# Attention and two MLP stages on one core: the seven-sum form of the second product in 19 of 24 blocks

## What is computed

```
q_n, k_n = rmsnorm(q, g_q), rmsnorm(k, g_k)
attn = softmax(q_n @ k_n^T / sqrt(64));  x = (attn @ v) as (4, 448, 768)
xn = (x - mean) / sqrt(var + 1e-6) * g_ln
x = x + relu(xn @ w_ch1) @ w_ch2             # first MLP
u = x + (x^T @ U @ V)^T                      # mixing over the sequence, rank 32
out = u + relu(u @ w_ch1b) @ w_ch2b          # second MLP
```

## Time and profile before

| | before |
|---|---|
| median of 3 runs | 1674.16 us |
| the profiled execution | 1675.43 us, span 1673.6 us |
| granted TensorE clock, mean | 0.998 |
| TensorE matmul busy | 98% of the span, 9878 instructions |
| VectorE, ScalarE, GpSimd busy | 68%, 44%, 29% |
| DMA | 43% of 16 engines' time, 146 GB/s |

### The profile page before, as it was taken

One profiled execution on the slowest core, in us unless ns is written; L12 is line 12 of the kernel. 1 busy time (PEld: TensorE's weight loads), 2 busy tenths in 40 slices (PEclk: granted clock), 3 DMA queues, 4 the chain that ended last, 5 costly groups with the idle time before them and its releaser, 6 DMA issues.

```text
span 1673.6 us, 27323 instructions
## 1 busy us (share of the span) xinstructions
PE 1632.0 (98%) x9878; PEld 1452.8 (87%) x9878; DVE 1140.2 (68%) x1934; ACT 736.8 (44%) x1637; POOL 482.8 (29%) x426
## 2 busy tenths in 40 slices
PE   9999988899999999999999999999999999999998
PEld 7766666688999999998899999999999899999998
DVE  6877788865556558838766787556645783766667
ACT  5777887852333224413433343323323431443333
POOL 5666777811111114201220132111111330122211
PEclk9999999999999999999999999999999999999999
DMA  4223333223555356452355355445535754234541
GB/s 124 73 66 89 88 121 117 84 86 116 183 179 188 126 193 215 167 192 93 129 181 185 121 190 186 164 143 175 186 122 179 254 188 150 81 123 161 170 169 68
DMA packets 92308, 243.68 MB, mean 146 GB/s; under 512 B 10160, under 2 KB 41008, under 8 KB 92176
## 3 DMA queue, kind: packets, MB, share of 16 engines
q1 hardware_dynamic: 92176, 241.94, 43.3%
HBM read 162.07 MB, written 79.82 MB: 145 GB/s over the span
## 4 chain that ended last, share of the span: by engine, by line
PE 78%; DVE 2%; ACT 1%; DMA 1%; issue 1%; SPq 0%; DVEq 0%; ACTq 0%
PE mm_ps L1002 35%; PE mm_ps L1021 26%; PE mm_ps L1011 12%; PE mm_ps L956 1%; PE sc_ps L1033 1%; PE sc_ps L1043 1%; PE sc_ps L943 1%; PE mm_ps L935 1%; PE sc_ps L977 1%; DMA w_kept<-w_hl 0%; DVE acc L1432 0%; PE sc_ps L1051 0%; ACT e_t L1120 0%; DVE h_lo L1396 0%; DVE w_hl L1360 0%
## 5 line engine op out<-in xcount | busy, mean ns | idle before, releaser
L1002 PE MATMUL mm_ps<-in_hi,w_hl 128*128 128x448 f32 x2016 | 589.5, 368 | 1.2 <-DVE ht L1417 1.1
L1021 PE MATMUL mm_ps<-h_hi,w_hl 128*128 128x448 f32 x1440 | 417.2, 367 | 0.0
L1002 PEld LDWEIGHTS mm_ps<-in_hi,w_hl 128*128 128x128 f32 x2016 | 379.0, 188 | 32.3 <-issue 2.0
L1002 PE MATMUL mm_ps<-in_lo,w_hl 128*128 128x448 f32 x1008 | 368.9, 366 | 0.0
L1021 PEld LDWEIGHTS mm_ps<-h_hi,w_hl 128*128 128x128 f32 x1440 | 270.7, 188 | 22.4
L1021 PE MATMUL mm_ps<-h_lo,w_hl 128*128 128x448 f32 x720 | 263.7, 366 | 0.0
L1157 ACT ACTIVATE w_hl<-w_raw 128x384 fp32r<-128x384 f32 (+1 forms) x382 | 173.1, 469 | 157.1 <-PE mm_ps L1021 78.0
L1441 DVE TENSOR_TENSOR acc<-mm_ps,acc 128x448 f32<-128x448 f32 x180 | 103.8, 618 | 201.0 <-PE mm_ps L1021 200.9
L1011 PE MATMUL mm_ps<-h_hi,w_hl 128*128 128x448 f32 x756 | 220.9, 367 | 0.5 <-issue 0.5
L1002 PEld LDWEIGHTS mm_ps<-in_lo,w_hl 128*128 128x128 f32 x1008 | 189.7, 188 | 14.7
L1360 DVE TENSOR_TENSOR w_hl<-w_raw,w_hl 128x384 fp32r<-128x384 f32 (+1 forms) x382 | 194.3, 517 | 5.0 <-ACT w_hl L1157 4.5
(11 more groups left out here) (119 smaller groups left out, 2289.1 us busy)
## 6 DMA issues: line engine op xcount, KB each, us to landing
w_raw<-in_w SPq DMA_DIRECT2D x76, 768.0 KB, 5.4
w_kept<-w_hl SPq DMA_DIRECT2D x140, 384.0 KB, 6.3
w_hl<-w_kept SPq DMA_DIRECT2D x140, 384.0 KB, 3.9
qk<-in_qkv SPq DMA_DIRECT2D x23, 448.0 KB, 4.1
acc<-xres SPq DMA_DIRECT2D x6, 1344.0 KB, 9.8
qt_raw<-in_q_t SPq DMA_DIRECT2D x24, 224.0 KB, 2.9
v<-in_qkv SPq DMA_DIRECT2D x24, 224.0 KB, 2.6
xnrm<-st_n SPq DMA_DIRECT2D x24, 224.0 KB, 2.0
```

The source lines that it names most:

```text
L1002: last = nc.tensor.matmul(bank(q), w[a][:, c * P:(c + 1) * P], x[:, k, c], start=k not in ONTO and c == 0 and p == 0, stop=c == HC - 1 and ...
L1021: last = nc.tensor.matmul(bank(q, b), w[a][:, c * P:(c + 1) * P], x[:, half, 2 * c + b], start=half == 0 and c == 0 and p == 0, stop=half ...
```

## The change

1. `by_sums` becomes true in 19 blocks: `SUMS_FROM = (2, 0, 0, 0)`, that is j = 2 to 4 of stage 0, j = 0 to 4 of stages 1 and 2, and j = 0 to 5 of stage 3. Which groups' weights are stored and fetched (`FIRST_KEPT = 1`) stays, so in the 10 added blocks the first product's weights are split in the block itself.
2. A third buffer `w_raw2`, used from block 2 of stage 0 on (its first load stands at product 42); buffers are taken in turn.
3. The differences for P7 and P4 move from VectorE to GpSimd (`later_sum`, with the semaphore `sub2_done`); that of P7 stands at m0 + 1 instead of m0 + 2.
4. Positions: G weights are split 4 instead of 3 products ahead from group 2 of stage 0; S weights 6 ahead where the block's groups are fetched, 5 where they are split; the sums of weights move along. P2 is split at m0 + 6 and P4 at m0 + 9. Stores of split weights stand 3 products earlier in the DMA queue's order.
5. Mixing: one item per 24 products in both stages, the same offsets for both. Inputs of a next stage are loaded at -13, -8 and 2 in all stages.

```diff
-    FIRST_KEPT, FLIP = 1, 0
+    FIRST_KEPT, SUMS_FROM, THIRD_FROM = 1, (2, 0, 0, 0), 42
     def by_sums(s, j):
-        return s % 2 == 1 and FIRST_KEPT <= j and (s == STAGES - 1 or j < NJ - 1)
+        return SUMS_FROM[s] <= j and (s == STAGES - 1 or j < NJ - 1)
...
-        high_at.setdefault(q - (7 if kind == "S" else 4), []).append(q)
-        low_at.setdefault(q - (6 if kind == "S" else 3), []).append(q)
+        low_lead[q] = 4 if kind == "G" and q >= number["G", 0, 2, P1] else 3 if kind != "S" else 6 if kept(number["G", s, 2 * n, P1]) else 5
+        high_at.setdefault(q - low_lead[q] - 1, []).append(q)
+        low_at.setdefault(q - low_lead[q], []).append(q)
...
-            sums_at.setdefault(number["G", s, n, P1] + {P5: -5, P7: -5, P6: -4, P3: 0}[k], []).append(q)
+            sums_at.setdefault(number["G", s, n, P1] + {P5: -5, P7: -5, P6: -4, P3: 0}[k] + 3 - low_lead[q], []).append(q)
         if kind == "S" and k[0] in (P5, P7, P6, P3):
-            sums_at.setdefault(q - {P5: 11, P7: 16, P6: 9, P3: 9}[k[0]], []).append(q)
+            first = {P5: 11, P7: 16, P6: 9, P3: 9} if low_lead[q] == 6 else {P5: 9, P7: 14, P6: 9, P3: 8}
+            sums_at.setdefault(q - first[k[0]], []).append(q)
...
+        third = run[0] >= number["G", 0, 2 * SUMS_FROM[0], P1]
+        x = min(range(2 + third), key=lambda x: loaded[x][-1:] or [-1])
...
-                                (P7, m0 + 2, m0 + 4), (P2, None, m0 + 5), (P4, m0 + 6, m0 + 8)):
+                                (P7, m0 + 1, m0 + 4), (P2, None, m0 + 6), (P4, m0 + 6, m0 + 9)):
...
-    MIX_FROM, MIX_STEP, ITEMS = 4, {1: 23, 2: 22}, 2 * HC
+    MIX_FROM, MIX_STEP, ITEMS = 4, 24, 2 * HC
...
+                def later_sum(s, j, k):
+                    g = s * NG + 2 * j
+                    if k == P7:
+                        rectified(pool, g + 1, C12)
+                        cut(pool, "f", s, j, P5)
+                        in0, in1 = relu_pair(g + 1, SECOND), relu_pair(g, SECOND)
+                    if k == P4:
+                        rectified(pool, g + 1, C21)
+                        cut(pool, "f", s, j, P6)
+                        in0, in1 = relu_pair(g + 1, FIRST), sub_pair(P6)
+                    nc.gpsimd.tensor_tensor(sub_pair(k), in0, in1, ALU.subtract).then_inc(sub2_done, 1)
...
-                        if stored(n):
-                            store_split(n)
+                        if n + 3 < Q and stored(n + 3):
+                            store_split(n + 3)
```

More of the change, by code:

```diff
@@ L103, in planned @@
         at = dict(zip(ks, at))[k[0] if kind == "S" else k]
-        at = at if j % 2 == FLIP else (at + 3) % 6
+        if j == SUMS_FROM[s] and kind == "G" and n % 2 == 0 and k == P1:
+            flip[s] = j % 2 if free.index(0) < free.index(3) else 1 - j % 2
+        at = at if j % 2 == flip[s] else (at + 3) % 6
         return [at + d for d in range(HC)] if kind == "S" else [at]
     banks, before = {}, {}
-    free, last_use = list(range(6)), {}
+    free, last_use, flip = list(range(6)), {}, {}
     for q, (kind, s, n, k) in enumerate(prods):
@@ L168, in mixer_kernel @@
             sums_at[at].sort(key=lambda q: (P5, P7, P6, P3).index(prods[q][3]))
-    for r, run in enumerate(runs[2:], 2):
+    raw_at, raw_before, raw_no, loaded = [], [], [], [[], [], []]
+    for r, run in enumerate(runs):
         kind, s, n, k = prods[run[0]]
-        if kind != "G" and s % 2 == 1 and n >= FIRST_KEPT:
-            at = number["G", s, 2 * n, P7 if run[0] in (number.get(("S", s, n, (P5, 0))), number.get(("M", s, n, 6))) else P1]
-        else:
-            at = runs[r - 2][-1] - 2
-        load_at.setdefault(at, []).append(r)
+        third = run[0] >= number["G", 0, 2 * SUMS_FROM[0], P1]
+        x = min(range(2 + third), key=lambda x: loaded[x][-1:] or [-1])
+        raw_at.append(x)
+        raw_before.append(loaded[x][-1] if loaded[x] else None)
+        loaded[x].append(r)
+        raw_no.append(len(loaded[x]))
+        if r < 2:
+            continue
+        if raw_before[r] is None:
+            at = THIRD_FROM
+        elif kind != "G" and kept(number["G", s, 2 * n, P1]):
+            first = run[0] in (number.get(("S", s, n, (P1, 0))), number.get(("M", s, n, 0)))
+            at = number["G", s, 2 * n, P1 if first else P7]
+        else:
+            at = runs[raw_before[r]][-1]
+            at = at - low_lead[at] + 1
+        load_at.setdefault(max(at, *load_at) if load_at else at, []).append(r)
     sum_no = {}
@@ L268, in mixer_kernel @@
             for tile in range(4):
[L269 to L272 removed]
+                load_made_at.setdefault(("prod", first + (-13, -8, 2)[c]), []).append((s, c, tile))
+    MIX_FROM, MIX_STEP, ITEMS = 4, 24, 2 * HC
     def mix_of(q):
         s = prods[q][1]
[L276 removed]
+        if s not in (1, 2) or q >= number["M", s, NJ - 1, 0]:
             return None
[L278 removed]
+        m, off = divmod(q - number["G", s, 0, 0] - MIX_FROM, MIX_STEP)
         if not 0 <= m < ITEMS:
@@ L607, in load_weights @@
                 def load_weights(r):
-                    if r >= 2:
-                        split(sp, runs[r - 2][-1])
+                    if raw_before[r] is not None:
+                        split(sp, runs[raw_before[r]][-1])
+                    elif r >= 2:
+                        for i in range(2):
+                            sp.wait_ge(xn_out[i], 8 * NP_)
                     kind, s, n, k = prods[runs[r][0]]
@@ L839, in weight_sum @@
                     weights_in(pool, r)
-                    a11, a12, a21, a22 = (w_raw[r % 2][:, n] for n in range(4))
+                    a11, a12, a21, a22 = (w_raw[raw_at[r]][:, n] for n in range(4))
                     p5, p6 = product_of(r, P5), product_of(r, P6)
@@ L1035, in mixing @@
                         last.then_inc(z_done, 1)
-                    i, part = divmod(off - 4 + mix_late(item), 3)
+                    i, part = divmod(off - 3, 3)
                     if 0 <= i < NI and part == 0:
@@ L1200, in hidden_relu @@
                             all_made(act, s + 1)
+                        if s == 0:
+                            for i in range(2):
+                                act.wait_ge(xn_out[i], 8 * NP_)
                     if g % 2 == 1 and h == C11:
@@ L1217, in mixing @@
                 def mixing(item, off):
-                    i, part = divmod(off - 5 + mix_late(item), 3)
+                    i, part = divmod(off - 4, 3)
                     if 0 <= i < NI and part == 0:
@@ L1443, in mixing @@
                 def mixing(item, off):
-                    i, part = divmod(off - 6 + mix_late(item), 3)
+                    i, part = divmod(off - 5, 3)
                     if 0 <= i < NI and part == 0:
```

63 lines of the change are left out of this document (32 added, 31 removed).

## The result

| | before | changed |
|---|---|---|
| median | 1674.33 us (7 runs, 1673.72 to 1680.89) | 1666.82 us (7 runs, 1662.10 to 1672.50) |
| ratio, 95% interval | | 0.9944 (0.9922 to 0.9966) |
| profiled execution, span | 1675.43, 1673.6 us | 1672.50, 1670.5 us |

The change gains 7.5 us of the 36.5 that the fewer matmuls are worth. The forecast was 1658; the measured time lies 8.8 us above it, inside the range, and a hair above what was called faster (1665.8).

A forecast was written before the change was run, and what follows sets the result against it. TensorE's matmul count was taken as the bound in every block. 1675.4 - 36.5 + 18 + 1 - 1.6 + 2 = 1658.3, less 1.3 is 1657; the forecast median was 1658 us, range 1637 to 1677.

The forecast's parts named there:

- The bound and the fewer matmuls: TensorE's matmul count bounds every block; ten blocks lose 18 matmuls each, 3.65 us a block, 36.5 us in all.
- The stops in the new blocks: GpSimd's sums and P7 difference hold VectorE up; P6 starts 1.8 us late, ten blocks 18 us, range 0 to 32.
- rival A: The forecast itself: new blocks give back about half their gain, 1.2 to 2.7 us each; 1650 to 1666, chance 0.42.
- the wait at P6: In new blocks, P6 at position 4 starts 1.8 us late, which includes P3 of g1 waiting for P5's combine.
- GpSimd's difference: The P7 difference, new on GpSimd, was taken as 2.0 us, between 1.7 and 2.4, holding VectorE up 1.8.
- The rule on the shared port: VectorE and GpSimd exclude each other on SBUF; taken literally, holding lasts the whole duration, giving a time near 1671.
- The pace: After stops, matmuls may run at 206.7 instead of 202.7 ns; 2 us more, upper end 24 us.
- The old blocks: In the nine old blocks, GpSimd's P7 difference delays VectorE; 1 us put for all, at most 9.
- Mixing: TensorE's wait for an item's tile, 1.4 us, and 0.2 beside it go with a step of 24 products: -1.6 us.
- B: Rival: collisions are covered by VectorE's waits for TensorE, lateness under 1.2 us; 1636 to 1650, chance 0.28.
- C: Rival: holding is the whole duration, 3.2 us a block, or a late load or store; 1671, chance 0.22.

The follow-up runs named there:

- thin_sums: Changed kernel with GpSimd's eight weight sums in the ten new blocks cut to 8 elements a row instead of 384; 1645.59 us, ratio 0.9823.
- own_scratch: Changed kernel with a separate scratch tile for the weight sums of the second product's second half; 1657.40 us, ratio 0.9892; run again, 1657.59 us.
- diff_p7_p4_dve: Changed kernel with the P7 and P4 differences moved back from GpSimd to VectorE; 1665.04 us, ratio 0.9938.
- scratch_p7_dve: own_scratch with only the P7 difference back on VectorE, the P4 one left on GpSimd; 1660.05 us, ratio 0.9909.

## Why the prediction was right or wrong

**The bound and the fewer matmuls: right.** 180 matmuls went. thin_sums, where nearly all else is unchanged, ran 29 us below before.

**The stops in the new blocks: the cause right, the size 5 us too small.** Ten blocks at 1.8 us of lateness, 18, were forecast. The records show 18.0 of idle time, but idle time is not the lateness (below): by the distance of starts TensorE lost 23.1 us in them, 2.3 a block, inside rival A's 1.2 to 2.7. That the two 18s agree is chance. The chain begins where it was put: GpSimd starts 4.2 us into g1 (3.8 forecast), takes turns with VectorE, and the combine of P5 is late. thin_sums shows the cause, own_scratch the part of it that is their place. Two things in the walk were wrong. Most of the delay falls at position -2, 1.45 of 2.08 us, where it was named as a part of the wait at P6. And VectorE did not catch up by P7: 0.38 us stand there, and they go with the P4 difference on GpSimd. The per-block value is a mean of unlike numbers, 0.65 to 2.9.

**GpSimd's difference: right.** 2.0 us were taken, between rows at 1.7 and 2.4; the median of 38 is 2.13 (from the changed kernel's records of L895):

```profile
L895 POOL TENSOR_TENSOR make_a<-make_b,make_a x38: 2089/2128/2977, 488.9 to 1646.0; 128x896 f32<-128x896 f32 x38
```

The prediction has no sum for its move alone; diff_p7_p4_dve and scratch_p7_dve put that within 3 us either way.

**The rule on the shared port.** The Trainium skill, "SBUF — State Buffer", section "Who interferes with whom", would have the whole duration as holding, a lateness of 3.2 us a block and a time near 1671. The block shown, without mixing, lost 2.8 us by the distance of starts, the ten 2.3 in the mean, between the 1.8 from the row's 0.88 of a sum and the 3.2; the runs do not decide which holding is right. In kind the rule agrees, as the 1.90 us for P5's low part shows.

**What a stop costs.** A stop costs more than its recorded idle time. Over the 1.45 us stop, matmul starts are 537.99 and 539.80, 1.81 apart instead of 0.20, and the next start follows after 0.28: 1.7 us lost for 1.45 recorded. The other stops of this trace show 0.12 to 0.25 us more than recorded, most of them 0.24, so 29 more stops are some 7 us. Where the records say 18.0 us for the new blocks and 3.0 for the old ones, TensorE lost 23.1 and 5.4.

**The pace: mis-sized.** I put 2 us for more of the time at 206.7 ns. By the distances of the low-part matmuls, 19% of the regular runs were slow before, 44% in the first trace of the changed kernel, 34% in the second. Of 6100 matmuls, at 4 ns each, that is 4 to 6 us more. The distances themselves, summed, give 4.7 us more in the first trace and 2.8 in the second. Which share is the change's and which chance stays open. It carries much of the spread: stage 3 took 315.8 us in the first trace and 313.0 in the second.

**The old blocks: 1 us forecast, 2.3 of recorded idle time found.** Their stops went from 0.7 to 3.0 us, by the distance of starts from 1.3 to 5.4; five are the 0.16 to 0.18 us of stage 3, which come only at the slow pace.

**Mixing: -1.6 forecast, -0.9 found.** The wait for the item's tile fell from 1.39 to 0.54 us; a wait of 0.42 for another one (L1071) is new. A stop of 0.89 us in the last block of stage 2, which no term had, went.

**The sum again.** For the first trace, from stage 0's first product to the last: -36.5, +19.0 of recorded stops, +7 of their surplus, +6 of pace, +1.6 of the clock (below): -2.9, where 3.9 us were gained. The median of all runs is 7.5 us better than before. Against the 1658.3 that the prediction's sum gave for a profiled execution, this one is 14.2 us longer. Some 13 of them are found: about 5 in the stops of the new blocks, 3 in those of the old ones, 3 in the pace, 1.6 in the clock, and the rest small. The terms that were too small are thus the price of the new blocks' stops, that of the old blocks', and the pace; the mechanism was the forecast one.

Rival A was the case by what the traces show, though the time, 1666.8, lies 0.8 us above its end of 1666. B fell in the traces. C's time (1671) is nearer to the measured one than the forecast is, but its reason, 3.2 us a block or a late load, was not found. By the prediction's own threshold of 0.5% the outcome is, by a hair, no difference, to which it gave 0.22, and not "faster", to which it gave 0.70.

## What to carry over

When TensorE is full and the sum of its work falls, read the densest ten microseconds of the engine that feeds it, not its mean load: here the 12 us of room a block that the sum left VectorE were no help, since eight GpSimd instructions came together with it. Ask of each helper what lets it start; a scratch tile of 1.5 KB a partition gave back 10 us. Price a stop by the distance of starts, not by the recorded idle time.

## What the hardware showed beside

**Two paces at one granted clock.** Runs of 128x448 matmuls go at 202.7 or at 206.7 ns each. The windows show the granted clock at 1.00 at either pace. Counted over the starts of all twelve traces, in runs of 18 matmuls or more, the pace turned 258 times. In 250 of them the turn stands at a break, that is at a distance of starts above 0.215 us or at another matmul (an item of the mixing, a pair). Only 8 lie inside an unbroken run, four in each direction, and five of these within 5 us behind a stop. Which pace follows is not set by the break: the slow pace followed 123 of 661 breaks that came at the quick pace and 49 of 176 that came at the slow one. Why there are two paces, and what picks one, was not found.

**A drop of the clock after a stop of 2.0 us.** In stage 2's block 4, TensorE stood from 1260.2 to 1262.2. Windows of the changed kernel (us; PE, PEld, DVE, ACT, POOL busy; granted clock; DMA):

```profile
1255.00:1262.00 7.00, 5.23 (x26) 4.51 (x24) 6.97 (x9) 1.53 (x3) 6.36 (x6) 1.00 0.91 288
1262.00:1265.00 3.00, 2.78 (x9) 2.51 (x10) 1.50 (x3) 1.83 (x4) 2.51 (x3) 0.63 0.42 159
1265.00:1268.00 3.00, 3.00 (x14) 2.74 (x13) 1.38 (x3) 0.99 (x2) 1.54 (x2) 0.80 0.03 5
```

For some 3 us the clock was at its lower level, 1.2 GHz, and 18 matmuls took 5.45 us instead of 3.88. own_scratch had the same drop in one trace and not in the other, behind the same stop; the second trace of the changed kernel had the stop and no drop. In the twelve traces there are 15 stops of 2.0 to 2.3 us behind the attention, and six of them were followed by such a drop of 3.4 us; none of the shorter stops there, up to 1.47 us, was.
